# VectorE's order around the low half of h: ahead of the routing table, and ahead of the scaling of the tile before

## The chip, the core and the metric

The kernel runs on one core of a Trainium2 chip. The time is the device time of one execution in microseconds (us). Five engines work side by side, each through its own list of instructions in order: TensorE (PE in the profile; its weight loads are PEld), VectorE (DVE), ScalarE (ACT), GpSimd (POOL) and SyncE (SP). They wait for each other on semaphores only. A queue named with a q (SPq, DVEq, POOLq) is the part of an engine that handles registers, branches, waits and the start of transfers.

## What is computed

A retention layer, a gated feed-forward layer, and a mixture of experts with one expert per token. What matters here is the third:

```
logits = x @ w_gate;  e_idx = argmax(logits)
gate_w = softmax(logits)[e_idx];  eom = sigmoid(x @ w_output_gate)
for each expert e:
    h  = relu(x[rows of e] @ w1[e])
    ye = h @ w2[e]
    out[rows of e] = gate_w * eom[:, e] * ye
```

There are 3072 tokens of width 512, 8 experts and 1024 hidden columns in an expert. All matrices are float32. Each float32 product is made of three products in a shorter format: a factor is split into a high part (a cast) and a low part (the value less its high part), and high by high, high by low and low by high are added up.

## The kernel before

The tokens are sorted by expert into tiles of 128 rows. Tile 0 and tile 1 run with expert 0 while the sorting goes on; from tile 2 on, the order comes from a table (`tile_tab`) that VectorE writes in `dve_route`. Which expert a tile uses, and whether the next one changes it, is read from that table into registers. In this data 27 tiles run, 0 to 26, and the expert changes 7 times.

One tile i goes like this, with the names of the code:

- GpSimd gathers its 128 rows into `xg` by an indirect DMA (`gather`, L1367), from indices in `idx_gather`.
- PE transposes them (`x_T`, L663) into bank 4. VectorE splits the result into high and low (`split_xe`, L675 and L677) and copies the rows' scale (`keep_scale`, L667, semaphore `scale_kept`).
- PE multiplies by w1 (`up`, L1427, 24 matmuls) into banks 0 and 1; ScalarE applies the relu (L1293).
- PE transposes h (`h_T`, L1435) into banks 2 and 3, in two halves. ScalarE casts each half to `hT_hi` (L1298, semaphore `hT_hi_done`). VectorE computes `hT_lo`, in two halves too (`hT_rest`, L1162, semaphore `hT_lo_done`).
- PE multiplies by w2 (`down`, L1451, 24 matmuls in 8 groups of three) into bank 5 or 6 by turns. It may start when half 0 of `hT_lo` is there, needs half 1 in the middle, and needs that bank free (`ye_read` of the tile two before).
- VectorE scales the rows into `ye` (`scale_y`, L1332), and GpSimd scatters them to the output (`scatter`, L1372). `scale_y` waits for the end of the `down` of its tile (`ye_done`) and for a free half of `ye` (`ye_free`).

PE's order is skewed: h_T(i), up(i+1), x_T(i+2), down(i), h_T(i+1), and so on. So the low part of tile i is wanted only after an `up`, save at two places where there is no `up` between them:

- Tile 1, during the routing. PE's order is down(0), the first half of the sort (`pe_sort`, L1153), the rest of down(0), h_T(1), the second half of the sort (semaphore `slots_done`), down(1). The `x_T` of tile 2 stands inside down(1), ahead of its last group of three.
- The last tile, 26. PE's order is down(25), with h_T(26) inside, then at once down(26). The low and high parts of this tile have buffers of their own (`hT_last`).

VectorE's loop over the tiles is in pairs. In `in_pairs` pairs 1 to 11 run in a loop, and the rest (pairs 12 to 15) in a second loop, where each pair stands under a test (`pairs > m`). With 13 pairs in this data the last three are skipped, and VectorE's queue goes through the loop's registers and branches for them (L1252, L1253).

When a tile changes the expert, ScalarE and VectorE also split the new weights (`split_w1` and `split_w2`, L700 and L703). SyncE loads them (L721): it may start when the table is written (`route_done`) and when GpSimd has asked for the gathers of tiles 2, 3 and 4 (`rows_asked`). The gather of tile 4 waits for `scale_kept` of tile 2, since it writes to the same buffer.

Of the kernel before, what the change touches and what calls it, by code (L numbers as in the profile page):

```python
# [88 lines left out]
def build(nc, steps_in, weights_in, gates_in, w1_in, w2_in, const_in, xT_dram, x_dram, out):  # L89
# [12 lines left out]
    def place(name, shape, dt=F32, where=None):  # L102

        offset = at[0] if where is None else where
        t = nc.alloc_sbuf_tensor_at(name, list(shape), dt, offset=offset)
        after = (offset + int(np.prod(shape[1:])) * 4 + 31) // 32 * 32
        assert after <= nc.sbuf_usable_end, (name, after)
        if where is None:
            at[0] = after
        return t.ap()  # L110
# [114 lines left out]
    hT_hi = place("hT_hi", (P, KE, P), F32R)  # L225
# [5 lines left out]
    hT_lo = place("hT_lo", (P, KE, P), F32R)  # L231
# [422 lines left out]
    ye_done, ye_read, ye_free, last_ye = sem("ye_done"), sem("ye_read"), sem("ye_free"), sem("last_ye")  # L654
# [14 lines left out]
    def split_xe(dve, i, s):  # L669
        dve.wait_ge(xe_T_done, i + 1)  # L670
        if isinstance(i, int) and i < FIRST:
            keep_scale(i, xg_first[s])
        at_bank = {0: 3, 1: 2}.get(i, 4) if isinstance(i, int) else 4
        psum = bank[at_bank].rearrange("p (k t) -> p k t", k=KD)
        nc.vector.tensor_copy(xe_hi[:, s], psum).then_inc(xe_done, 1)  # L675
        dve.wait_ge(xe_done, 2 * i + 1)
        nc.vector.tensor_tensor(xe_lo[:, s], psum, xe_hi[:, s].bitcast(F32), ALU.subtract).then_inc(xe_done, 1)  # L677
        if not (isinstance(i, int) and i < FIRST):
            keep_scale(i, xg[s])
# [28 lines left out]
    def split_w2(eng, hi, run, parts=range(PARTS)):  # L708
        split_weight(eng, hi, run, raw2, raw2_in, w2_hi, w2_lo, W2_SPAN, w2_hi_done, w2_lo_done, parts)
# [112 lines left out]
    def on_pe(g):  # L822
        return g - (GROUPS - 2)
# [33 lines left out]
    def dve_partial(dve, g, part=part_sb):  # L857
        dve.wait_ge(part_done, on_pe(g) + 1)
        nc.vector.tensor_copy(part, apart(g)).then_inc(part_read, 1)
# [20 lines left out]
    def linker(dve, base, link_done=link_done):  # L880

        count = [0]

        def link(ins):
            count[0] += 1
            ins.then_inc(link_done, 1)
            dve.wait_ge(link_done, base + count[0])

        return link, count
# [265 lines left out]
        if half == 1:  # L1155
            ins.then_inc(slots_done, 1)

    def hT_rest(dve, i, hT=(hT_hi, hT_lo)):
        high, low = hT
        for o in range(2):  # L1160
            dve.wait_ge(hT_hi_done, 2 * i + o + 1)
            nc.vector.tensor_tensor(low[:, 4 * o:4 * o + 4].rearrange("p k t -> p (k t)"), bank[2 + o],  # L1162
                                    high[:, 4 * o:4 * o + 4].rearrange("p k t -> p (k t)").bitcast(F32),
                                    ALU.subtract).then_inc(hT_lo_done, 1)

    def dve_route(dve):
        v = nc.vector
        known = LAST * TG
        link, count = linker(dve, LINKED)
        split_w2(dve, False, 0, (0, 1))  # L1170
        split_xe(dve, 1, 1)
        for t in range(TG):
            dve.wait_ge(yT_done, TG * on_pe(LAST) + t + 1)
            v.tensor_copy(yT_last[:, :, t * P:(t + 1) * P], bank[4 + t].rearrange("p (k t) -> p k t", k=KD)).then_inc(yT_read, 1)
        split_w2(dve, False, 0, (2,))
        dve_partial(dve, LAST, part_last)
        split_w2(dve, False, 0, (3,))
        dve_logits(dve, LAST)
        dve_choose(dve, LAST, link)
        dve_gate(dve, LAST, link)  # L1180
        dve_scale(dve, LAST, link)
        hT_rest(dve, 0)

        dve.wait_ge(rank_done, GROUPS)
        link(v.tensor_scalar(e_cnti, bank[7][:, COUNT:COUNT + NE], float(P - 1), None, ALU.add))
        link(v.tensor_scalar(e_tli, e_cnti, 7, None, ALU.logical_shift_right))
        link(v.tensor_copy(e_tiles, e_tli))
        src = e_tiles
        for dst, shift in ((e_s1, 1), (e_s2, 2), (e_end, 4)):
            v.tensor_copy(dst[:, 0:shift], src[:, 0:shift])  # L1190
            link(v.tensor_tensor(dst[:, shift:], src[:, shift:], src[:, 0:NE - shift], ALU.add))
            src = dst
        link(v.tensor_tensor(e_base, e_end, e_tiles, ALU.subtract))
        dve_rank(dve, LAST, link)

        dve_off_hot(dve, known, TILES)
        link(v.tensor_tensor(base8, onehot, under(e_base, TILES), ALU.mult))
        link(v.tensor_reduce(t_base, base8, AX.X, ALU.add))
        link(v.tensor_tensor(t_base, t_base, t_tle, ALU.add))

        link(v.tensor_tensor(tile_eq, under(iota[:, 0:COLS], TILES), over(t_base, COLS), ALU.is_equal))
        v.tensor_tensor(tile_hot, tile_eq, over(id1, COLS), ALU.mult).then_inc(hot_done, 1)

        v.tensor_scalar(e_used, e_tiles, 0.0, None, ALU.is_gt)
        link(v.tensor_scalar(e_s1[:, 0:1], e_end[:, NE - 1:NE], -1.0, None, ALU.add))
        link(v.tensor_scalar(tl_i, iota[:, 0:COLS + 1], e_s1[:, 0:1], None, ALU.min))
        link(v.tensor_tensor(tl_cmp, under(e_end, COLS + 1), over(tl_i, NE), ALU.is_le))
        link(v.tensor_tensor(tl_cmp2, tl_cmp, under(e_used, COLS + 1), ALU.mult))

        dve.wait_ge(slots_done, 1)  # L1210
        v.tensor_scalar(idx_gather[:, FIRST:], bank[7][:, FIRST:COLS], -1.0, 0.0, ALU.add, ALU.max).then_inc(gather_ready, 1)
        v.tensor_copy(inv, bank[7][:, 0:COLS])

        v.tensor_reduce(tl_e, tl_cmp, AX.X, ALU.add)
        link(v.tensor_reduce(tl_run, tl_cmp2, AX.X, ALU.add))
        link(v.tensor_tensor(tl_new, tl_run[:, 1:COLS + 1], tl_run[:, 0:COLS], ALU.subtract))

        dve.wait_ge(x_out, 16 * GROUPS)
        link(v.tensor_copy(pair_i, e_end[:, NE - 1:NE]))
        v.tensor_scalar(n_pairs, pair_i, 1, None, ALU.logical_shift_right)  # L1220
        v.tensor_copy(tile_tab[:, :, 0], tl_e[:, 0:COLS])
        v.tensor_copy(tile_tab[:, :, 1], tl_run[:, 0:COLS])
        v.memset(tile_tab[:, 0:1, 2], 1)
        v.tensor_copy(tile_tab[:, 1:COLS, 2], tl_new[:, 0:COLS - 1])
        v.tensor_copy(tile_tab[:, :, 3], tl_new).then_inc(route_done, 1)

        hT_rest(dve, 1)
        v.tensor_scalar(inv_e, inv, 0.0, float(2 * NT), ALU.is_equal, ALU.mult)
        link(v.tensor_scalar(inv_s, inv, -1.0, None, ALU.add))
        link(v.tensor_tensor(inv_s, inv_s, inv_e, ALU.add))  # L1230
        link(v.tensor_copy(idx_scatter, inv_s))
        last = dve.value_load(n_pairs[0:1, 0:1], min_val=PAIRS_MIN, max_val=PAIRS_MAX)
        v.tensor_scalar(n_before, n_pairs, -1, None, ALU.add)
        v.tensor_copy(idx_last, idx_scatter[:, bass.ds(last * 2, 1)]).then_inc(scatter_ready, 1)
# [93 lines left out]
    def dve_experts(dve):  # L1328
        def scale_y(i, s):
            dve.wait_ge(ye_done, i + 1)  # L1330
            dve.wait_ge(ye_free, i - 1 + 2)
            return nc.vector.tensor_scalar(ye[:, s], bank[5 + s], slot_scale[:, bass.ds(i, 1)], None, ALU.mult)  # L1332

        def tile(i, s):
            with dve.If(entry(dve, i, NEW_NEXT) == 1):
                split_w1(dve, False, entry(dve, i, RUN) + 1)
            if not isinstance(i, int):
                split_xe(dve, i + 1, 1 - s)
            with dve.If(entry(dve, i, NEW_HERE) == 1):
                split_w2(dve, False, entry(dve, i, RUN))  # L1340
            scale_y(i - 1, 1 - s).then_inc(ye_read, 1)

        def pair(m):
            hT_rest(dve, 2 * m)
            tile(2 * m + 1, 1)
            hT_rest(dve, 2 * m + 1)
            tile(2 * m + 2, 0)

        split_xe_early(dve, 2, 0)
        split_xe(dve, 3, 1)  # L1350
        with dve.If(entry(dve, 1, NEW_NEXT) == 1):
            split_w1(dve, False, 1)
        scale_y(0, 0).then_inc(ye_read, 1)
        tile(2, 0)
        pairs = dve.value_load(n_pairs[0:1, 0:1], min_val=PAIRS_MIN, max_val=PAIRS_MAX)
        in_pairs(dve, pairs, pair)
        hT_rest(dve, pairs * 2, hT_last)
        scale_y(pairs * 2, 0).then_inc(last_ye, 1)


# [216 lines left out]
```

## Time and profile before

| | us |
|---|---|
| median of 3 runs | 1047.63 (1045.71 to 1048.64) |
| the profiled execution | 1046.8, its span 1045.0 |
| PE busy | 1017.6 (97% of the span) |
| VectorE busy | 554.5 (53%) |
| ScalarE busy | 283.6 (27%) |
| GpSimd busy | 112.4 (11%) |
| share of PE in the chain that ended last | 96% |

The span is the time from the first to the last instruction of the profiled execution; 1.8 us of its time lie around the span. The granted clock is the share of TensorE's full clock that it was given: 1.00 stands for 2.4 GHz and 0.50 for 1.2 GHz.

### The profile page before, as it was taken

How to read it: one execution, taken by the hardware profiler on the slowest of the kernel's cores; microseconds unless marked ns; L12 is line 12 of the kernel's file. 1: busy time of each engine (PE TensorE's matmuls, PEld its weight loads, DVE VectorE, ACT ScalarE, POOL GpSimd, SP SyncE). 2: the span in 40 equal slices, each digit the busy share in tenths (PEclk: the TensorE clock that was granted, in tenths of full speed). 3: DMA queues.
4: the chain of work that ended last, by engine and by line, in shares of the span. 5: the costliest groups of instructions: out<-in, count | busy, mean ns of one | idle time of the engine just before them, and what ended most of it. 6: DMA issues, size and time to landing. Idle time of an engine off the chain costs nothing.

```text
span 1045.0 us, 17350 instructions
## 1 busy us (share of the span) xinstructions
PE 1017.6 (97%) x5761; PEld 844.9 (81%) x5762; DVE 554.5 (53%) x1211; ACT 283.6 (27%) x490; POOL 112.4 (11%) x108
## 2 busy tenths in 40 slices
PE   6989999999999999999999999998999999999996
PEld 5878888888888888888888878887888888888885
DVE  3444333487557747773877223474554545445541
ACT  2534332221112122112211212130534433334330
POOL 4780000000000000000000000001121111111111
PEclk9999999999999999999999999999999999999999
DMA  9998800511051114104210212011753435253311
GB/s 364 368 295 249 223 1 1 139 53 48 4 151 51 41 34 129 53 28 99 73 51 21 81 41 81 11 51 42 281 193 133 144 105 167 74 192 120 118 36 36
DMA packets 53874, 114.50 MB, mean 110 GB/s; under 512 B 8750, under 2 KB 23406, under 8 KB 53297
## 3 DMA queue, kind: packets, MB, share of 16 engines
q1 hardware_dynamic: 48752, 98.95, 30.1%
q0 software_dynamic: 4480, 13.91, 4.0%
q8 instruction: 38, 0.62, 0.2%
q10 hardware_dynamic: 576, 0.79, 0.2%
q14 instruction: 28, 0.22, 0.1%
HBM read 96.81 MB, written 17.61 MB: 109 GB/s over the span
## 4 chain that ended last, share of the span: by engine, by line
PE 96%; DMA 2%; issue 1%; DVE 1%; ACT 0%; POOL 0%; ACTq 0%; DVEq 0%; POOLq 0%
PE bank L1077 38%; PE bank L1097 19%; PE bank L1427 15%; PE bank L1451 14%; PE bank L1435 2%; PE bank L604 2%; PE bank L555 2%; PE bank L663 1%; PE bank L569 1%; PE bank L590 1%; DMA rows<-in_steps 1%; DMA qdec_t<-in_consts 1%; PE bank L1153 0%; PE bank L977 0%; PE bank L844 0%
## 5 line engine op out<-in xcount | busy, mean ns | idle before, releaser
L1077 PE MATMUL bank<-x_hi,wab_hi 128*128 128x512 f32 x576 | 224.4, 390 | 0.0
L1077 PE MATMUL bank<-x_hi,wab_lo 128*128 128x512 f32 x576 | 224.1, 389 | 0.0
L1077 PE MATMUL bank<-x_lo,wab_hi 128*128 128x512 f32 x576 | 224.1, 389 | 0.0
L999 DVE SCALAR_TENSOR_TENSOR products<-y_sb,gate_row 128x512 f32<-128x512 f32 x256 | 176.8, 691 | 22.7 <-DMA gate_row<-xT_dram 15.3
L1427 PE MATMUL bank<-w,xe 128*128 (+1 forms) x648 | 158.9, 399 | 0.5 <-DVE xe L687 0.5
L1011 DVE TENSOR_TENSOR g_sb<-bank,b_sb 128x512 f32<-128x512 f32 x72 | 49.7, 690 | 175.3 <-PE bank L1077 175.3
L1427 PEld LDWEIGHTS bank<-w,xe 128*128 128x128 f32 x648 | 119.3, 188 | 28.2 <-issue 1.8
L1077 PEld LDWEIGHTS bank<-x_hi,wab_hi 128*128 128x128 f32 x576 | 108.1, 188 | 22.7 <-issue 0.2
L1077 PEld LDWEIGHTS bank<-x_hi,wab_lo 128*128 128x128 f32 x576 | 108.1, 188 | 22.4
L1077 PEld LDWEIGHTS bank<-x_lo,wab_hi 128*128 128x128 f32 x576 | 108.2, 188 | 22.3
L1097 PE MATMUL bank<-wo_hi,g_hi 128*128 128x512 f32 x288 | 113.4, 394 | 0.0
L1097 PE MATMUL bank<-wo_hi,g_lo 128*128 128x512 f32 x288 | 112.2, 390 | 0.0
L1097 PE MATMUL bank<-wo_lo,g_hi 128*128 128x512 f32 x288 | 112.1, 389 | 0.0
L789 ACT CAST g_hi<-g_sb 128x512 fp32r<-128x512 f32 x72 | 44.7, 621 | 231.0 <-DVE g_sb L1011 231.0
L787 ACT COPY b_sb<-bank 128x512 f32<-128x512 f32 x72 | 42.3, 587 | 214.1 <-PE bank L1077 214.1
L1367 POOL DMA_INDIRECT xg<-x_rows,idx_gather x28 | 29.2, 1043 | 649.8 <-DVE idx_gather L969 597.7
L1451 PE MATMUL bank<-w_hi,hT_hi 128*128 (+1 forms) x208 | 84.3, 405 | 2.8 <-DVE hT_lo L1162 2.8
L1451 PE MATMUL bank<-w_hi,hT_lo 128*128 (+1 forms) x208 | 82.0, 394 | 0.0
L1451 PE MATMUL bank<-w_lo,hT_hi 128*128 (+1 forms) x208 | 81.6, 393 | 0.0
L1013 DVE TENSOR_TENSOR g_lo<-g_sb,g_hi 128x512 fp32r<-128x512 f32 x72 | 49.8, 692 | 49.5 <-ACT g_hi L789 49.5
L1097 PEld LDWEIGHTS bank<-wo_hi,g_hi 128*128 128x128 f32 x288 | 54.1, 188 | 11.7 <-issue 0.8
L1097 PEld LDWEIGHTS bank<-wo_hi,g_lo 128*128 128x128 f32 x288 | 54.1, 188 | 11.5
(172 smaller groups left out, 1052.7 us busy)
## 6 DMA issues: line engine op xcount, KB each, us to landing
raw<-in_w SPq DMA_DIRECT2D x64, 512.0 KB, 7.9
gate_row<-xT_dram SPq DMA_DIRECT2D x64, 256.0 KB, 3.2
rows<-in_steps SPq DMA_DIRECT2D x20, 768.0 KB, 8.3
rows<-in_steps SPq DMA_DIRECT2D x24, 256.0 KB, 7.6
wab_raw<-in_weights SPq DMA_DIRECT2D x24, 256.0 KB, 9.0
x_rows<-y_sb SPq DMA_DIRECT2D x6, 1024.0 KB, 8.6
xT_dram<-x_all SPq DMA_DIRECT2D x4, 1024.0 KB, 11.5
x_raw<-xT_dram SPq DMA_DIRECT2D x16, 256.0 KB, 8.0
```

Source lines behind the costliest of these rows:

```text
L555: ins = nc.tensor.matmul(bank[2 * i + o][:, cols], kT[half_p, cols], qT[half_p, cols], start=True, stop=True)
L604: ins = nc.tensor.matmul(out_at(i, p, o), rows[:, c, 3, h * D:(h + 1) * D], probs[j][:, i, h, :], start=False, stop=(i == ROUND - 1 and p ...
L787: nc.scalar.copy(b_sb[:, f % 2], b_bank(f)).then_inc(b_read, 1)
L789: nc.scalar.copy(g_hi[:, f % 2], g_sb[:, f % 2]).then_inc(g_hi_done, 1)
L999: nc.vector.scalar_tensor_tensor(products, y_sb[:, t], 1.0, gate_row[e % GATE_SLOTS], ALU.mult, ALU.mult, accum_out=L3[:, t, e:e + 1]).the ...
L1011: nc.vector.tensor_tensor(g_sb[:, f % 2], a_bank(f), b_sb[:, f % 2], ALU.mult).then_inc(g_done, 1)
L1013: nc.vector.tensor_tensor(g_lo[:, f % 2], g_sb[:, f % 2], g_hi[:, f % 2].bitcast(F32), ALU.subtract).then_inc(g_lo_done, 1)
L1077: ins = nc.tensor.matmul(to, wab(w, f, j), x[s][:, k, :], start=(k == 0 and m == 0), stop=(k == KD - 1 and m == 2))
L1097: ins = nc.tensor.matmul(bank[4 + t], gp[:, f % 2, toks], wo(w, f), start=(f == 0 and m == 0), stop=(f == KF - 1 and m == 2))
L1367: nc.gpsimd.indirect_dma_start(out=xg_first[s] if i < FIRST else xg[s], out_offset=None, in_=x_rows[0:rows_there], in_offset=bass.Indirect ...
L1427: ins = nc.tensor.matmul(bank[o], x[:, s, k, :], w[:, bass.ds(half + (k * FE + o * 512), 512)], start=(k == 0 and m == 0), stop=(k == KD - ...
L1451: ins = nc.tensor.matmul(bank[5 + s], h[:, k, :], w[:, bass.ds(half + k * DM, DM)], start=(k == 0 and m == 0), stop=(k == KE - 1 and m == 2))
```

## The change

Nothing is added and nothing taken out: two kinds of instruction take another place in VectorE's list. In the routing, the two halves of `hT_rest` of tile 1 stood behind the last write of the table. Half 0 now stands ahead of the wait for the sort (`slots_done`), and half 1 right behind the instruction that writes `idx_gather`. In the expert loop `scale_y(i - 1)` was the last step of `tile(i)`, so it stood ahead of `hT_rest` of tile i. Now it stands behind it, and ahead of the splits of the tile after. The last two scalings follow the last `hT_rest`.

```diff
-    def hT_rest(dve, i, hT=(hT_hi, hT_lo)):
+    def hT_rest(dve, i, hT=(hT_hi, hT_lo), halves=range(2)):
         high, low = hT
-        for o in range(2):
+        for o in halves:
...
+        hT_rest(dve, 1, halves=(0,))
         dve.wait_ge(slots_done, 1)
         v.tensor_scalar(idx_gather[:, FIRST:], bank[7][:, FIRST:COLS], -1.0, 0.0, ALU.add, ALU.max).then_inc(gather_ready, 1)
+        hT_rest(dve, 1, halves=(1,))
         v.tensor_copy(inv, bank[7][:, 0:COLS])
...
         v.tensor_copy(tile_tab[:, :, 3], tl_new).then_inc(route_done, 1)
 
-        hT_rest(dve, 1)
         v.tensor_scalar(inv_e, inv, 0.0, float(2 * NT), ALU.is_equal, ALU.mult)
...
             with dve.If(entry(dve, i, NEW_HERE) == 1):
                 split_w2(dve, False, entry(dve, i, RUN))
-            scale_y(i - 1, 1 - s).then_inc(ye_read, 1)
 
         def pair(m):
             hT_rest(dve, 2 * m)
+            scale_y(2 * m - 1, 1).then_inc(ye_read, 1)
             tile(2 * m + 1, 1)
             hT_rest(dve, 2 * m + 1)
+            scale_y(2 * m, 0).then_inc(ye_read, 1)
             tile(2 * m + 2, 0)
...
         in_pairs(dve, pairs, pair)
         hT_rest(dve, pairs * 2, hT_last)
+        scale_y(pairs * 2 - 1, 1).then_inc(ye_read, 1)
         scale_y(pairs * 2, 0).then_inc(last_ye, 1)
```

VectorE's list around the sort, before the change. L1208 is the last step that needs nothing from the sort, L1211 writes the gather's indices, L1225 is the last write of the table, L1228 begins the scatter's indices:

```order
L1208 TENSOR_TENSOR tl8_1_158<-tl8_0_157,e_5_80 128x280 [waits link_done]
L1211 TENSOR_SCALAR idx_gather_52<-bank7 128x32 [waits slots_done,link_done]
L1212 COPY inv_0_150<-bank7 128x34
...
L1225 CAST tile_tab_136<-inv_3_153 128x34
L1162 TENSOR_TENSOR hT_lo_133<-bank2,hT_hi_131 128x512 [waits hT_hi_done]
L1162 TENSOR_TENSOR hT_lo_133<-bank3,hT_hi_131 128x512 [waits hT_hi_done]
L1228 TENSOR_SCALAR inv_1_151<-inv_0_150 128x34
```

The same place after the change (L1212 now writes the gather's indices, L1227 is the last write of the table):

```order
L1208 TENSOR_TENSOR tl8_1_158<-tl8_0_157,e_5_80 128x280 [waits link_done]
L1162 TENSOR_TENSOR hT_lo_133<-bank2,hT_hi_131 128x512 [waits hT_hi_done,link_done]
L1212 TENSOR_SCALAR idx_gather_52<-bank7 128x32 [waits slots_done]
L1162 TENSOR_TENSOR hT_lo_133<-bank3,hT_hi_131 128x512 [waits hT_hi_done]
L1214 COPY inv_0_150<-bank7 128x34
...
L1227 CAST tile_tab_136<-inv_3_153 128x34
L1229 TENSOR_SCALAR inv_1_151<-inv_0_150 128x34
```

One half passes the whole table and the wait for the sort; the other stays behind the index write and passes the rest of the table.

The end of VectorE's list before the change. Bank 6 holds the result of tile 25 and bank 5 that of tile 26; L1253 and L1252 are the loop over pairs:

```order
L1332 REGISTER_ALU [waits ye_free,ye_done]
L1332 TENSOR_SCALAR ye_134<-bank6,slot_scale_54 128x512
L1253 UNCONDITIONAL_BRANCH
L1252 REGISTER_ALU
L1252 COMPARE_AND_BRANCH
L1161 ISA
L1162 TENSOR_TENSOR hT_last_lo_145<-bank2,hT_last_hi_144 128x512 [waits hT_hi_done]
L1161 REGISTER_ALU
L1162 TENSOR_TENSOR hT_last_lo_145<-bank3,hT_last_hi_144 128x512 [waits hT_hi_done]
```

And after it:

```order
L1253 REGISTER_ALU
L1253 COMPARE_AND_BRANCH
L1161 ISA
L1162 TENSOR_TENSOR hT_last_lo_145<-bank2,hT_last_hi_144 128x512 [waits hT_hi_done]
L1161 REGISTER_ALU
L1162 TENSOR_TENSOR hT_last_lo_145<-bank3,hT_last_hi_144 128x512 [waits hT_hi_done]
L1333 ISA [waits ye_free,ye_done]
L1333 TENSOR_SCALAR ye_134<-bank6,slot_scale_54 128x512
```

The loop's branches and the low part of the last tile no longer stand behind the wait for the end of down(25).

## Rows read from the trace of the kernel before

**Rows 1.** Waits of PE from 600 us on: us in total, times, longest.

```profile
PE bank L1451 <- DVE hT_last_lo L1162: 3.5, 1, 3.5
PE bank L1451 <- DVE hT_lo L1162: 2.8, 1, 2.8
```

**Rows 2.** Timeline around down(1): start us, duration us, instruction, [idle before, releaser].

```profile
711.26 1.07 ACT L1298 CAST hT_hi<-bank 128x512 fp32r<-128x512 f32 x2 [6.67 <-PE bank L1435]
...
713.02 0.19 DVE L1211 TENSOR_SCALAR idx_gather<-bank 128x32 int32<-128x32 f32 x1 [3.46 <-PE bank L1153]
...
714.05 0.99 POOL L1367 DMA_INDIRECT xg<-x_rows,idx_gather  x1 [35.55 <-DVE idx_gather L1211]
...
714.92 0.68 DVE L1162 TENSOR_TENSOR hT_lo<-bank,hT_hi 128x512 fp32r<-128x512 f32 x1
...
715.35 1.00 POOL L1367 DMA_INDIRECT xg<-x_rows,idx_gather  x1 [0.31 <-issue]
...
715.66 0.50 PE L1451 MATMUL bank<-w_hi,hT_hi 128*128 128x512 f32 x1 [2.75 <-DVE hT_lo L1162]
...
722.14 0.60 PE L663 MATMUL bank<-ident,xg 128*128 128x128 f32 x4
...
723.97 2.37 PE L1427 MATMUL bank<-w,xe 128*128 x9 [0.53 <-DVE xe L687]
```

**Rows 3.** Timeline of one tile of the loop whose successor changes the expert.

```profile
805.20 0.75 DVE L1332 TENSOR_SCALAR ye<-bank,slot_scale 128x512 f32<-128x512 f32 x1 [4.11 <-PE bank L1451]
805.54 1.07 ACT L1298 CAST hT_hi<-bank 128x512 fp32r<-128x512 f32 x2 [5.77 <-PE bank L1435]
...
806.16 1.29 DVE L1162 TENSOR_TENSOR hT_lo<-bank,hT_hi 128x512 fp32r<-128x512 f32 x2 [0.21 <-ACT hT_hi L1298]
...
808.96 4.63 DVE L703 TENSOR_TENSOR w<-raw,w 128x1024 f32 x4 [1.51 <-ACT w L700]
...
811.73 0.48 PE L1451 MATMUL bank<-w_hi,hT_hi 128*128 x1
...
814.23 0.69 DVE L677 TENSOR_TENSOR xe<-bank,xe 128x512 fp32r<-128x512 f32 x1
...
817.29 1.04 PE L1435 MATMUL bank<-ident,h_sb 128*128 128x128 f32 x8
```

**Rows 4.** Busy time, clock and DMA by stretch: PE, PEld, DVE, ACT, POOL, PEclk, DMA share, GB/s.

```profile
717.00:719.00 2.00, 2.00 (x6) 1.52 (x6) 0.29 (x2) 0.00 (x0) 0.00 (x0) 0.50 0.48 129
```

**Rows 5.** The gather of tile 2, from its issue at 714.05: median us to landing.

```profile
xg<-x_rows,idx_gather POOLq DMA_INDIRECT x1, 3.4
```

**Rows 6.** Timeline of the gather of tile 4, the first weight loads, and up(4).

```profile
725.30 1.00 POOL L1367 DMA_INDIRECT xg<-x_rows,idx_gather  x1 [8.95 <-DVE slot_scale L667]
...
729.30 4.76 SPq L721 DMA_DIRECT2D raw<-in_w  x8
...
741.66 0.69 DVE L677 TENSOR_TENSOR xe<-bank,xe 128x512 fp32r<-128x512 f32 x1
...
743.77 5.85 PE L1427 MATMUL bank<-w,xe 128*128 x24
```

**Rows 7.** Timeline of the end, from the last h_T on.

```profile
1026.74 1.07 ACT L1298 CAST hT_last_hi<-bank 128x512 fp32r<-128x512 f32 x2 [4.00 <-PE bank L1435]
...
1028.82 0.40 PE L1451 MATMUL bank<-w_hi,hT_lo 128*128 x1
...
1029.35 0.75 DVE L1332 TENSOR_SCALAR ye<-bank,slot_scale 128x512 f32<-128x512 f32 x1 [5.30 <-PE bank L1451]
...
1031.70 1.29 DVE L1162 TENSOR_TENSOR hT_last_lo<-bank,hT_last_hi 128x512 fp32r<-128x512 f32 x2 [1.60 <-issue]
...
1032.77 0.49 PE L1451 MATMUL bank<-w_hi,hT_last_hi 128*128 x1 [3.55 <-DVE hT_last_lo L1162]
...
1039.72 0.39 PE L1451 MATMUL bank<-w_hi,hT_last_lo 128*128 x1
```

**Rows 8.** Busy time, clock and DMA of one stretch of down(26).

```profile
1034.00:1037.00 3.00, 3.00 (x9) 2.32 (x8) 0.00 (x0) 0.00 (x0) 0.00 (x0) 0.50 0.00 0
```

## The prediction

> **What bounds the kernel now.** I read the chain that ended last first: 96% of it is PE, so only what lets PE start earlier, or run faster, is worth time. Then the waits of PE in the expert part: two of them are on the low part of h, 3.5 us at the last tile and 2.8 us at tile 1 [rows 1]. Then the timelines around these two, to see what VectorE did meanwhile, and the granted clock behind each. The reader is to see that in both places VectorE has the low part standing behind something that it doesn't need: behind the routing table at tile 1 [rows 2], behind the end of down(25) and the loop's branches at tile 26 [rows 7]. In the loop proper PE waits for nothing.
>
> **Place 1, tile 1.** Before, the sort ends at 712.91 (715.66 less the idle 2.75), and PE waits for half 0 of the low part, which runs from 714.92 to 715.60 [rows 2].
> After, half 0 needs only ScalarE's first cast. In the loop the low part starts 0.62 after the pair of casts (805.54 to 806.16) [rows 3]; the pair begins here at 711.26 [rows 2], so half 0 runs from 711.88 to 712.56. VectorE is idle then (3.46 us up to 713.02), so the index write stays at 713.02 and the gather at 714.05. Half 1 follows at about 713.13 and is there at 713.8, while PE wants it 12 matmuls in, near 715.5. Half 0 is there some 0.3 us before the sort ends; down(1) follows the sort, and the stall of 2.75 goes.
> A second term is the clock. In down(1) it stands at 0.50 (1.2 GHz) in the stretch read [rows 4], behind a stall of 2.75. Its 21 matmuls up to x_T(2) take 722.14 - 715.66 = 6.48 us. At full clock 24 take 817.29 - 811.73 = 5.56 [rows 3], 0.23 each, so 21 take 4.87. That is 1.61 saved if PE, now not idle, keeps 2.4 GHz.
> What is late next: x_T(2) would stand at 712.91 + 4.87 = 717.78, by the ends, or some 0.2 earlier, since matmuls overlap. The gather of tile 2 lands 3.4 us behind 714.05, at 717.45 [rows 2, 5]. That is just in time; between nothing and 0.3 us are lost there, and I take 0.1. Place 1 gives 2.75 + 0.2 (overlap) + 1.61 - 0.1 = 4.5 us.
> What follows has to come forward too. The table is written 0.6 us later than before, by one low half (half 1) ahead of it (713.13 to 713.8), but PE, SyncE and ScalarE want it only behind x_T(2). The scatter's indices come 0.6 us earlier, as half 0 now lies in the idle time. The weight loads begin at 729.30, behind the gather of tile 4 at 725.30, which itself waited 8.95 us for the scale of tile 2 [rows 6]. That chain starts from x_T(2), so it shifts with PE. With it goes the tightest margin I found, up(4): its x is split until 741.66 + 0.69 = 742.35, and PE starts at 743.77, 1.4 us later [rows 6]. The margin stays 1.4 if both move.
>
> **Place 2, the last tile.** Before, VectorE waits for the end of down(25), scales at 1029.35, goes through the branches of three skipped pairs, and starts the low part at 1031.70; PE starts down(26) at 1032.77 [rows 7]. After, VectorE's last step ends at 1024.05 (1029.35 less its idle 5.30). The branches take at most 1031.70 - 1029.35 = 2.35 us, and the table load ahead of them at most 0.75 (the idle 1.51 ahead of a split of w1 holds two of them [rows 3]), so its queue is through by 1027.15. ScalarE's casts begin at 1026.74, so half 0 may start at 1027.36 and ends at 1028.04. Down(25)'s last matmul starts at 1028.82, so down(26) can start one step (0.23) later, at 1029.05: 1032.77 - 1029.05 = 3.72 us.
> The clock again: 0.50 in the middle of down(26) [rows 8]. First to last matmul takes 1039.72 - 1032.77 = 6.95; at full clock 23 steps of 5.56/24 are 5.33. That saves 1.62. The scaling of tile 25 still starts at 1029.35, when down(25) ends, with nothing ahead of it; its scatter is out long before the last one. Place 2 gives 3.72 + 1.62 = 5.3 us, and all of it reaches the end, since behind down(26) stand only one scaling and one scatter.
>
> **The loop.** In the loop's tiles `scale_y` goes behind the low part. VectorE waited there for the end of down, and then for ScalarE's cast by another 0.21 [rows 3], so the low part does not come earlier, and the scaling comes some 2.2 us later (807.4 for 805.2). Behind it stands the split of w1, ahead of which VectorE is idle for 1.51, part of that with register work of its own [rows 3]: I put its delay at 0.2, and at 0.75 (the whole scaling) at most. The x split behind it ends at 814.92 and the next up starts behind the transposes of 817.29, 2.4 us later or more: covered. The scatter goes 2.2 us later, and behind it a gather that PE wants more than a tile later; a tile is 12.1 us (805.20 to 817.29): covered. Bank 5 or 6 is wanted again two tiles on. I put the loop at 0, between 0.2 gained and 1 lost.
>
> **The sum.** 4.5 + 5.3 = 9.8 us. The profiled execution took 1046.8, so it would be 1037.0. The median of the runs is 0.8 above that execution: 1037.8.
>
> **Bounds.** Place 1: at least 2.75 - 0.5, if the clock falls anyway and x_T(2) waits half a microsecond; at most 4.7. Place 2: at least 3.55 (no gain of clock), at most 5.4. Sum between 5.8 and 10.1, plus or minus 1 for the median of three runs, which lay 2.9 apart.
>
> **A rule against it.** Gather 3 was issued at 715.35 and took GpSimd 1.00, while the low part ran on VectorE (714.92 to 716.2); gather 2 took 0.99 with only small steps beside it, and gather 4 at 725.30 took 1.00 [rows 2, 6]. So in this trace GpSimd does not wait for the low part. The Trainium skill ("SBUF — State Buffer", section "SBUF: two separate sides") says that VectorE and GpSimd share one pair of ports as an exclusive lock, and that a DMA issued by GpSimd can starve for descriptors while VectorE runs an operation that holds both. By that rule half 1, now at 713.1 to 713.8, could hold back gather 2; the trace does not agree, since the same operation beside gather 3 cost it 0.00 to 0.01.
>
> **Rivals.**
> *A. x_T(2) becomes the wait.* The gather's landing (717.45) and x_T(2) (717.6 to 717.8) are all but equal, and the index write or GpSimd's start may slip by up to one low half (0.68). PE then stands for up to 0.7, and with the wait of 0.53 before up(2) [rows 2] close behind, the clock may fall as it did before: 1.6 lost. Gain 9.8 - 0.7 - 1.6 = 7.5: 1040.1. For it: no margin. Against: nothing of before is ahead of the index write that is not idle time now.
> *B. The loads do not come forward.* If the first expert's weights hang on something else than tile 2's scale, PE comes 4.5 us early to up(4) with 1.4 of margin, waits 3.1, and loses 1.6 of clock: place 1 gives nothing, the sum is 5.3 to 5.1: 1042.4. Against: the 8.95 us wait of gather 4 on that scale [rows 6].
> *C. Slower.* The place is VectorE ahead of the w1 split in the 7 tiles that bring a new expert. If the scaling there had to wait for `ye_free` (its scatter two tiles before not landed), the split and the x split behind it would be late. From the point where this exceeds 2.4 us, up waits, say 0.5, each time with 1.6 of clock: 7 x (0.5 + 1.6) = 14.7, so 1037.8 + 14.7 = 1052.5. Against: the scalings shown waited for PE, 4.11 and 5.30 us, and not for a scatter [rows 3, 7]; the scatter now has 2.2 us less out of two tiles, 24.
> *D. Only one place works*, for instance the last low part is still late because VectorE's queue is: 9.8 less about 5 gives 1042.8.
>
> **How the numbers follow.** The forecast, both places whole: 0.72, 1037.8, by itself 1036.3 to 1039.3. A: 0.14. B: 0.05. C: 0.02. D: 0.05. Nothing changed at all: 0.02. A measurement of this kernel can tell about 0.3%, 3.1 us, from no change: faster means under 1044.5. The forecast, A, B and D lie below that, less a little for a mis-sized B or D: 0.95 faster, 0.035 same, 0.015 slower. The range reaches over A: 1035.8 to 1041.0.
>
> **What would show it.** Right: no wait of PE on a low part of h from 600 us on; granted clock 1.00 through down(1) and down(26); x_T(2) near 717.6 and the index write still near 713.0; weight loads starting near 724.8; down(26) starting one step behind down(25); the span 9.8 shorter, about 4.5 of it by 740 us. Wrong: a wait of PE at x_T(2) on the gather, or at up(4) on the weights; clock of 0.50 in either place; up waiting in the loop.

## The result and the profile after

The changed kernel takes 1037.36 us (median of 5 runs, 1037.05 to 1041.24), against 1047.63 of the kernel before (5 runs, 1045.71 to 1048.64). The ratio is 0.9914, with a 95% interval of 0.9893 to 0.9936: faster by 9.0 us, between 6.7 and 11.2. The ratio goes by all runs and not by the medians, which lie 10.3 apart. The profiled execution took 1037.36, its span is 1035.5. The forecast was 1037.8.

Waits of PE from 600 us on, kernel after:

```profile
PE bank L1430 <- DVE xe L687: 0.5, 1, 0.5
PE bank L1438 <- ACT h_sb L1294: 0.3, 1, 0.3
PE bank L1454 <- issue: 0.2, 1, 0.2
```

Both waits on a low part [rows 1] are gone. What is left is small: 0.5 at up(2), 0.3 at one h_T, and 0.2 on "issue", which is new.

Timeline of the kernel after around down(1) (start, duration, instruction, [idle before, releaser]):

```profile
711.60 1.07 ACT L1299 CAST hT_hi<-bank 128x512 fp32r<-128x512 f32 x2 [6.67 <-PE bank L1438]
711.76 1.49 PE L1153 MATMUL bank<-tile_hot,off_hot 128*128 128x34 f32 x12
712.29 0.69 DVE L1162 TENSOR_TENSOR hT_lo<-bank,hT_hi 128x512 fp32r<-128x512 f32 x1 [2.38 <-ACT hT_hi L1299]
713.10 0.48 PE L1454 MATMUL bank<-w_hi,hT_hi 128*128 128x512 f32 x1
713.29 0.19 DVE L1212 TENSOR_SCALAR idx_gather<-bank 128x32 int32<-128x32 f32 x1 [0.30 <-PE bank L1153]
713.40 0.68 DVE L1162 TENSOR_TENSOR hT_lo<-bank,hT_hi 128x512 fp32r<-128x512 f32 x1
...
714.33 0.99 POOL L1370 DMA_INDIRECT xg<-x_rows,idx_gather  x1 [35.45 <-DVE idx_gather L1212]
...
718.00 0.60 PE L663 MATMUL bank<-ident,xg 128*128 128x128 f32 x4
...
719.83 2.37 PE L1430 MATMUL bank<-w,xe 128*128 x9 [0.53 <-DVE xe L687]
...
721.16 1.00 POOL L1370 DMA_INDIRECT xg<-x_rows,idx_gather  x1 [4.53 <-DVE slot_scale L667]
...
725.15 4.67 SPq L721 DMA_DIRECT2D raw<-in_w  x8
```

Half 0 runs in what was idle time, down(1) follows the sort with no gap, and half 1 lies behind the index write, beside matmuls. The 21 matmuls up to x_T(2) take 718.00 - 713.10 = 4.90 us, for 6.48 before [rows 2]. The gather of tile 4 waits 4.53 for the scale of tile 2 instead of 8.95, and the weight loads begin at 725.15 for 729.30 [rows 6].

The end of the kernel after:

```profile
1022.75 1.08 ACT L1299 CAST hT_last_hi<-bank 128x512 fp32r<-128x512 f32 x2 [4.16 <-PE bank L1438]
...
1023.37 1.29 DVE L1162 TENSOR_TENSOR hT_last_lo<-bank,hT_last_hi 128x512 fp32r<-128x512 f32 x2 [3.46 <-ACT hT_last_hi L1299]
...
1024.84 0.40 PE L1454 MATMUL bank<-w_hi,hT_lo 128*128 x1
1025.07 0.39 PE L1454 MATMUL bank<-w_hi,hT_last_hi 128*128 x1
...
1025.38 0.75 DVE L1333 TENSOR_SCALAR ye<-bank,slot_scale 128x512 f32<-128x512 f32 x1 [0.72 <-PE bank L1454]
...
1030.29 0.39 PE L1454 MATMUL bank<-w_hi,hT_last_lo 128*128 x1
```

The low part starts 0.62 behind ScalarE's casts, as in the loop; down(26) starts 0.23 behind the last matmul of down(25) instead of 3.95 (1028.82 to 1032.77 [rows 7]). The clock in both places (columns as in rows 4):

```profile
713.00:718.00 5.00, 5.00 (x25) 4.08 (x25) 3.44 (x19) 0.00 (x0) 2.00 (x2) 1.00 0.30 74
1025.00:1030.00 5.00, 5.00 (x23) 4.13 (x23) 0.75 (x1) 0.00 (x0) 1.00 (x1) 1.00 0.14 52
```

It is 1.00 (2.4 GHz), where rows 4 and 8 had 0.50 (1.2 GHz).

**A ruler that leaves out the start.** Up to the second half of the sort all kernels of this study have the same instructions in the same order, and yet it starts anywhere from 709.77 to 712.77 in their traces. So I compare from its start (the L1153 row) to the end of the span: 1045.0 - 711.42 = 333.58 before, 1035.5 - 711.76 = 323.74 after. That is 9.84 us less, good to about 0.1, since the span is given to a tenth. It is made up of these pieces: from the sort to up(2) 12.55 before (711.42 to 723.97) and 8.07 after, 4.48 less; from the last matmul of down(25) to the last of down(26) 10.90 before and 5.45 after, 5.45 less; and about 0.1 is lost again between and behind them.

### The profile page after: what moved, and what is told of

It is laid out like the page before. It is cut to its first block, busy times and chain, and to the rows that moved or that the text cites. A ratio compares the mean times of both kernels' runs of the same rounds, so it can differ in the third digit from the quotient of the medians.

```text
span 1035.5 us, 17351 instructions
## 1 busy us (share of the span) xinstructions
PE 1014.7 (98%) x5761; PEld 843.4 (81%) x5762; DVE 553.4 (53%) x1211; ACT 283.6 (27%) x490; POOL 118.3 (11%) x108
## 4 chain that ended last, share of the span: by engine, by line
PE 96%; DMA 3%; issue 0%; POOL 0%; ACT 0%; DVE 0%; ACTq 0%; POOLq 0%; DVEq 0%
PE bank L1077 38%; PE bank L1097 19%; PE bank L1430 15%; PE bank L1454 14%; PE bank L1438 2%; DMA rows<-in_steps 2%; PE bank L604 2%; PE bank L555 2%; PE bank L663 1%; PE bank L569 1%; PE bank L590 1%; DMA qdec_t<-in_consts 1%; PE bank L1153 0%; PE bank L977 0%; PE bank L844 0%
## 5 line engine op out<-in xcount | busy, mean ns | idle before, releaser
L1370 POOL DMA_INDIRECT xg<-x_rows,idx_gather x28 | 35.1, 1252 | 646.2 <-DVE idx_gather L969 598.6
L1162 DVE TENSOR_TENSOR hT_lo<-bank,hT_hi 128x512 fp32r<-128x512 f32 x52 | 33.5, 685 | 73.7 <-ACT hT_hi L1299 73.7
```

The lines of the kernel that those rows point to most:

```text
L1370: nc.gpsimd.indirect_dma_start(out=xg_first[s] if i < FIRST else xg[s], out_offset=None, in_=x_rows[0:rows_there], in_offset=bass.Indirect ...
```

## The experiments

Four kernels split the change. A second set puts it under strain, and a third looks at what was left.

| kernel | median us | ratio to before (95%) | sort to end |
|---|---|---|---|
| before | 1047.63 | | 333.58 |
| after | 1037.36 | 0.9914 (0.9893 to 0.9936) | 323.74 |
| route_only | 1041.98 | 0.9952 (0.9939 to 0.9965) | 330.23 |
| loop_and_end | 1042.96 | 0.9958 (0.9942 to 0.9974) | 329.16 |
| end_only | 1041.44 | 0.9940 (0.9927 to 0.9953) | 328.99 |
| loop_only | 1043.48 | 0.9965 (0.9954 to 0.9977) | 330.47 |
| after_again | 1038.71 | 0.9917 (0.9899 to 0.9936) | 323.90 |
| route_and_end | 1036.62 | 0.9897 (0.9880 to 0.9914) | 323.54 |
| late_index | 1039.16 | 0.9913 (0.9893 to 0.9934) | 326.90 |
| loads_late | 1045.38 | 0.9976 (0.9959 to 0.9993) | 330.53 |
| load_early | 1036.31 | 0.9904 (0.9887 to 0.9922) | 323.32 |
| best | 1036.38 | 0.9903 (0.9888 to 0.9919) | 323.38 |
| both_ahead | 1037.31 | 0.9918 (0.9898 to 0.9938) | 323.81 |
| before_again | 1046.04 (one run) | | 333.08 |

The kernels route_only to loop_only ran on one chip, after_again to loads_late on a second, load_early to before_again on a third; each ratio is to the kernel before on the same chip. "Sort to end" is that of the one profiled execution of each.

### The change taken apart

**route_only**: the moves in `dve_route` alone.

```diff
+        hT_rest(dve, 1, halves=(0,))
         dve.wait_ge(slots_done, 1)
         v.tensor_scalar(idx_gather[:, FIRST:], ...)
+        hT_rest(dve, 1, halves=(1,))
...
-        hT_rest(dve, 1)
```

> Only the low part of tile 1 is moved (half 0 ahead of the wait for the sort, half 1 behind the index write); loop and end as before. Theory (the two places are separate, each gives its stall plus the loss of clock behind it): 4.1 to 4.5 us less than before, about 1043.2; no wait of PE at down(1), granted clock 1.00 there; the wait of 3.5 us at down(26) and the clock of 0.50 behind it as before. Rival (the places are not separate, or the end gives all of it): 0 to 2 us less.

Measured: 0.9952, 5.0 us less. From sort to up(2) 8.07 us (709.77 to 717.84), as in the kernel after. But sort to end is only 3.35 less than before, since the untouched end cost more this time: the same stall, and a longer slow stretch behind it. The end of route_only:

```profile
1022.65 0.40 PE L1452 MATMUL bank<-w_hi,hT_lo 128*128 x1
1026.60 0.79 PE L1452 MATMUL bank<-w_hi,hT_last_hi 128*128 x1 [3.55 <-DVE hT_last_lo L1162]
...
1034.75 0.39 PE L1452 MATMUL bank<-w_hi,hT_last_lo 128*128 x1
```

8.15 us from first to last matmul, for 6.95 before and 5.22 after. Place 1 is worth its 4.5 by itself.

**loop_and_end**: the moves in `dve_experts` alone; `hT_rest(dve, 1)` stands where it stood.

> The routing is as before; only the scaling is moved behind the low part, in the loop and at the end. Theory: 5.3 us less than before, about 1042.3; wait of 2.75 us at down(1) and clock 0.50 behind it as before; none at down(26). Rival (the gain at the end is only the stall, the clock falls all the same): 3.7 us less.

Measured: 0.9958, 4.4 us less. At the end 5.45 us, as in the kernel after (1030.52 to 1035.97). At down(1) the stall is 2.75 again, and its 21 matmuls take 7.33 us (716.28 to 723.61), for 6.48 before.

**end_only**: the loop keeps its old order; the new one only at the last pair of neighbours.

```diff
         def pair(m):
+            scale_y(2 * m - 1, 1).then_inc(ye_read, 1)
             hT_rest(dve, 2 * m)
             tile(2 * m + 1, 1)
+            scale_y(2 * m, 0).then_inc(ye_read, 1)
             hT_rest(dve, 2 * m + 1)
...
-            scale_y(i - 1, 1 - s).then_inc(ye_read, 1)
...
         hT_rest(dve, pairs * 2, hT_last)
+        scale_y(pairs * 2 - 1, 1).then_inc(ye_read, 1)
```

> The routing as before, the order in the loop as before (scaling of tile i-1 ahead of the low part of tile i), but the scaling of tile 25 behind the low part of tile 26: only the last pair of neighbours changes places. Theory (the loop's new order is worth nothing, the end is worth all): the same as loop_and_end within 0.3 us, 5.3 us less than before. Rival (the loop's order gives or costs something, by the split of w1 0.2 to 0.75 us later in 7 tiles, say): differs from loop_and_end by 1 us or more.

Measured: 0.9940, 6.3 us less; 5.45 at the end again (1029.35 to 1034.80). By the traces the loop's new order is worth nothing: sort to end is 0.17 less than in loop_and_end. The medians differ by 1.5, as the rival had it, but the two intervals overlap, and of the 1.17 between the two profiled executions (1041.88 and 1043.05) 1.03 lie ahead of the change, where the second half of the sort starts at 711.01 here and at 712.04 there.

**loop_only**: loop_and_end with the last two steps in the old order, so that only the branches of the skipped pairs come ahead.

```diff
-        hT_rest(dve, pairs * 2, hT_last)
         scale_y(pairs * 2 - 1, 1).then_inc(ye_read, 1)
+        hT_rest(dve, pairs * 2, hT_last)
         scale_y(pairs * 2, 0).then_inc(last_ye, 1)
```

> The routing as before; in the loop the scaling is behind the low part, but at the end the scaling of tile 25 stands ahead of the low part of tile 26, behind the loop's branches. Theory: the branches (2.35 us at most) are now done while PE works; the low part waits for the end of down(25), the scaling and ScalarE's cast that is long done, so PE's stall falls from 3.5 to about 1.5 us (scaling from 1029.35, low part 0.65 behind it, 0.7 long, 0.37 to PE). If the clock falls behind a stall of this length as it did behind 2.75 and 3.55, the gain is 2 us; if it does not, 2 + 1.6 = 3.6 us. Rival (the branches don't move, the whole gain came from the place of the scaling): no gain.

Measured: 0.9965, 3.7 us less. The end of loop_only, and the clock of two stretches behind the stall:

```profile
1028.86 0.75 DVE L1332 TENSOR_SCALAR ye<-bank,slot_scale 128x512 f32<-128x512 f32 x1 [5.54 <-PE bank L1453]
1029.53 1.28 DVE L1162 TENSOR_TENSOR hT_last_lo<-bank,hT_last_hi 128x512 fp32r<-128x512 f32 x2
...
1030.59 0.49 PE L1453 MATMUL bank<-w_hi,hT_last_hi 128*128 x1 [1.88 <-DVE hT_last_lo L1162]
...
1035.92 0.39 PE L1453 MATMUL bank<-w_hi,hT_last_lo 128*128 x1
```

```profile
1030.60:1033.00 2.40, 2.40 (x11) 1.99 (x12) 0.20 (x1) 0.00 (x0) 0.81 (x1) 1.00 0.29 109
1033.00:1036.00 3.00, 3.00 (x15) 2.42 (x13) 0.00 (x0) 0.00 (x0) 0.00 (x0) 1.00 0.00 0
```

The stall is 1.88, for about 1.5 expected, and the clock stays at 1.00: down(26) takes 5.33. So the 5.45 us of the end are, by these rows: 1.67 the branches (3.55 less 1.88), 2.05 the wait for the scaling and what it leads to (the rest of the 3.72), and 1.7 the clock (6.95 less 5.22).

### The change under strain

**after_again**: the kernel after, once more.

> The kernel after the change once more, beside the three below on one chip. About 1037.4; from the start of the second half of the sort (L1153) to the end of the span 323.7 us as in its first trace (before: 333.6).

Measured: 0.9917; sort to end 323.90, 0.16 from the first trace.

**late_index**: the index write later.

```diff
-        v.tensor_scalar(idx_gather[:, FIRST:], ...).then_inc(gather_ready, 1)
         hT_rest(dve, 1, halves=(1,))
         v.tensor_copy(inv, bank[7][:, 0:COLS])
         v.tensor_reduce(tl_e, tl_cmp, AX.X, ALU.add)
         link(v.tensor_reduce(tl_run, tl_cmp2, AX.X, ALU.add))
+        v.tensor_scalar(idx_gather[:, FIRST:], ...).then_inc(gather_ready, 1)
```

> The kernel after, with the write of idx_gather moved behind both low halves, the copy of inv and the two reductions, so 1.5 us later (714.8 for 713.3). Theory (x_T(2) in down(1) has a margin of 0.3 us on the gather of tile 2, which lands 3.3 us behind its issue): PE waits 1.1 to 1.3 us at x_T(2), and everything behind shifts by that; if the clock falls behind it, 1.6 to 2.8 us more, so 1038.6 or 1040.2 to 1041.4. Rival (the real margin is larger, the landing is earlier than the profile has it): under 0.5 us.

Measured: by its median no different from after_again, by the trace 3.0 us longer from sort to end (326.90 for 323.90). Timeline and clock of late_index:

```profile
710.80 1.49 PE L1153 MATMUL bank<-tile_hot,off_hot 128*128 128x34 f32 x12
...
713.86 0.19 DVE L1217 TENSOR_SCALAR idx_gather<-bank 128x32 int32<-128x32 f32 x1
714.90 1.00 POOL L1370 DMA_INDIRECT xg<-x_rows,idx_gather  x1 [37.00 <-DVE idx_gather L1217]
...
718.38 0.66 PE L663 MATMUL bank<-ident,xg 128*128 128x128 f32 x4 [1.18 <-DMA xg<-x_rows,idx_gather]
720.36 3.91 PE L1430 MATMUL bank<-w,xe 128*128 x9 [0.64 <-DVE xe L687]
```

```profile
718.40:720.30 1.90, 1.32 (x7) 0.85 (x7) 1.18 (x3) 0.00 (x0) 0.00 (x0) 1.00 0.29 112
720.40:724.00 3.60, 3.60 (x9) 2.89 (x10) 0.40 (x2) 0.00 (x0) 1.00 (x1) 0.53 0.17 34
```

The index write comes 3.06 behind the start of the sort's second half for 1.53 in the kernel after, 1.53 late; PE stands for 1.18 at x_T(2), so 0.35 of the delay does not show as idle time there. That is not free time, though: up(2) starts 9.56 behind the sort (720.36 less 710.80) for 8.07, 1.49 later, so it had a margin of 0.04 only. Behind the second wait, at up(2), the clock falls, and its first nine matmuls take 3.91 for 2.37. This is rival A as a kernel, with more than twice the 0.68 us of delay that A allows for: 1.49 + 1.54 = 3.0, all of it. The trace is of the slowest of its four executions (1039.54). Its granted clock was 0.998 over the whole span and 0.999 to 1.000 in the other three, so whether the clock fell behind up(2) in those too is open.

**both_ahead**: both low halves ahead of the wait for the sort (`hT_rest(dve, 1)` there, and nothing behind the index write).

> The kernel after, with both low halves of tile 1 ahead of the wait for the sort. Half 1 then runs from about 0.6 us behind half 0, and ends about 0.3 us behind the sort; the index write and the gather are 0.2 to 0.3 us later. Theory (margin at x_T(2) 0.3 us): PE waits 0 to 0.2 us there, the table is written 0.5 us earlier, which nothing needs; no difference from after. Rival (any delay of the index write reaches PE in full and pulls the clock down): 1.6 us or more slower.

Measured: 0.9918, sort to end 323.81. PE in both_ahead:

```profile
711.69 1.49 PE L1153 MATMUL bank<-tile_hot,off_hot 128*128 128x34 f32 x12
...
717.85 0.43 PEld L663 LDWEIGHTS bank<-ident,xg 128*128 128x128 f32 x4 [0.20 <-DMA xg<-x_rows,idx_gather]
...
719.93 2.35 PE L1429 MATMUL bank<-w,xe 128*128 x9 [0.72 <-DVE xe L687]
```

The index write is 0.21 later (1.74 behind the sort's start for 1.53), PE's weight load at x_T(2) waits 0.20 on the gather, and up(2) starts 8.24 behind the sort for 8.07, 0.17 later: again a margin of 0.04. By the end of the span this can't be told from the kernel after (323.74 and 323.90), so the place of half 1 is worth 0.2 us at most.

**loads_late**: SyncE is let loose behind the first scatter.

```diff
         gather(4)
-        pool.sem_inc(rows_asked, 1)
...
             scatter(1 - i % 2, idx_scatter[:, i - 1:i])
+            if i == 1:
+                pool.sem_inc(rows_asked, 1)
```

> The kernel after, but SyncE is let loose (rows_asked) only behind the scatter of tile 0, 4.8 us later (about 727.0 for 722.2). Nothing else moves. Theory (the first expert's weights have 1.4 us of margin at up(4), where x of tile 4 is split 738.2 and up(4) starts at 739.6, since both start from x_T(2)): up(4) is late by about 3.4 us, plus 1.6 to 2.8 if the clock falls; 1040.8 to 1043.6. Rival (the margin is much wider, the loads don't bound that split): no change.

Measured: 0.9976, only 2.5 us below the kernel before; sort to end 330.53, 6.8 more than after. PE in loads_late, and the x split of tile 4 on VectorE:

```profile
719.01 0.60 PE L663 MATMUL bank<-ident,xg 128*128 128x128 f32 x4
...
742.51 1.15 PE L1439 MATMUL bank<-ident,h_sb 128*128 128x128 f32 x8 [2.53 <-ACT h_sb L1294]
...
745.18 8.24 PE L1431 MATMUL bank<-w,xe 128*128 x24 [1.52 <-DVE xe L677]
```

```profile
744.04 0.69 DVE L677 TENSOR_TENSOR xe<-bank,xe 128x512 fp32r<-128x512 f32 x1
```

The first weight loads in loads_late, then up(4) in the kernel after (the view ends ahead of its last matmul):

```profile
731.25 14.40 SPq L721 DMA_DIRECT2D raw<-in_w  x12
```

```profile
739.62 5.61 PE L1430 MATMUL bank<-w,xe 128*128 x23
```

The x split of tile 4 ends 25.72 behind x_T(2) here (744.73 less 719.01) and 20.24 in the kernel after (738.24 less 718.00), 5.48 later; PE stands for 2.53 + 1.52 = 4.05, and up(4) starts 26.17 behind x_T(2) for 21.62, 4.55 later. So 0.93 us of the delay was free. The margin of 1.4 that the prediction and I read, from the end of the split to the start of up(4), is there (738.24 to 739.62), but 0.45 of it is what up(4) took to start behind the split even when it waited for it (744.73 to 745.18). The loads start 5.1 later, counted from x_T(2) (12.24 behind it for 7.15), near the 4.8 I had put down. The wait shows at two places, since ScalarE's relu of tile 3 is queued behind its weight casts, and h_T(3) waits for the relu. Up(4) then takes 8.24 for 5.85 [rows 6]. The median, 1045.38, lies above the 1040.8 to 1043.6 that I expected: the split was 0.7 later, and the margin 0.45 less, than I had reckoned with. This is rival B as a kernel, its loads 5.1 late where B has them 4.5 late: it took all of place 1 and more.

### What was left

**route_and_end**: route_only and end_only together.

> Both places of the change, but the loop keeps its old order (scaling of tile i-1, then the low part of tile i); only the scaling of tile 25 is behind the low part of tile 26. Theory (the loop's new order makes nothing faster; it moves GpSimd's gather 3 us later, onto PE's register load of n_before ahead of down(25), which then took 0.53 for 0.32 us and let PE stand 0.25): 0.1 to 0.3 us less than after_again from sort to end, 323.5; the load takes 0.32 again, its medians the same within noise. Rival (the 0.25 is chance): no difference, and the load is slow here too.

Measured: 0.9897; sort to end 323.54. The register load of PE (columns: count, min/median/max ns, start), first in route_and_end, then in the kernel after:

```profile
L1505 PEldq TENSOR_LOAD <-n_before x1: 322/322/322, 1015.3 to 1015.3; - x1
```

```profile
L1505 PEldq TENSOR_LOAD <-n_before x1: 537/537/537, 1017.1 to 1017.1; - x1
```

What lies around it in the kernel after:

```profile
1016.64 1.04 POOL L1370 DMA_INDIRECT xg<-x_rows,idx_gather  x1 [0.30 <-issue]
...
1018.59 0.49 PE L1454 MATMUL bank<-w_hi,hT_hi 128*128 x1 [0.20 <-issue]
```

In the five traces with the old loop order and the load at this place it takes 318 to 322 ns, in the seven with the new order 521 to 547. In the new order the scaling is later, with it GpSimd's scatter, and with that the gather behind it, which then lies on PE's load.

**load_early**: the kernel after with that load far ahead.

```diff
+        pe.wait_ge(scatter_ready, 1)
+        n_last = pe.value_load(n_before[0:1, 0:1], ...)
         to_next_pair(0, even, odd)
...
-        pe.wait_ge(scatter_ready, 1)
-        n = pe.value_load(n_before[0:1, 0:1], ...)
```

> The kernel after, with PE's register load of n_before (and its wait for scatter_ready) moved from ahead of down(25) to ahead of the first tiles of the loop, 300 us earlier, where PE's list is full. Theory (PE stood 0.20 to 0.26 us ahead of down(25) because this load took 0.53 us there beside GpSimd's gather): no wait ahead of down(25), from x_T(27) to down(25) 0.36 us as in the other tiles (0.80 in the kernel after, 0.64 before), sort to end 0.4 us less than after (323.4). Rival (the wait there is the loop's exit, not the load): 0.6 to 0.8 us stay.

Measured: 0.9904; sort to end 323.32, 0.42 less than after. PE ahead of down(25) in load_early:

```profile
1017.25 0.60 PE L663 MATMUL bank<-ident,xg 128*128 128x128 f32 x4
1017.60 0.49 PE L1454 MATMUL bank<-w_hi,hT_hi 128*128 x1
```

0.35 from x_T(27) to down(25), for 0.80 in the kernel after and 0.64 before. So the load did hold PE up there. That the gather beside it makes it slow is borne out by twelve traces, but not by a kernel in which the gather alone was moved.

**best**: route_and_end with the early load.

> route_and_end with the same early load: both places of the change, the loop's old order, the load out of the way. Theory: sort to end 323.3, the least of all; its median about 0.3 us below route_and_end, which is below what runs can tell, so 1036.5 to 1037.5. Rival (the load costs as much at its new place): as route_and_end.

Measured: 0.9903 (0.9888 to 0.9919), the same as load_early and route_and_end within their intervals; 323.38. The three can't be told apart, and none is shown to beat the kernel after.

**before_again**: a second trace of the kernel before.

> The kernel before once more, for a second trace of its two stalls. Theory (the stalls are fixed by the order, 2.75 and 3.55 us, but how long the clock stays at 0.50 behind each is not): stalls within 0.1 us of the first trace; the 21 matmuls of down(1) up to x_T(2) take 6.5 to 7.5 us (6.48 in the first trace), down(26) from its first to its last matmul 6.9 to 8.2 (6.95). Rival (the clock's loss is fixed by the stall): 6.48 and 6.95 again.

Measured: the stalls are 2.75 and 3.55 again, to the hundredth. Behind them the 21 matmuls take 6.25 (715.36 to 721.61) and down(26) 6.93: the first below the range I gave.

## Why the prediction was right, point by point

**What bounds.** Right: PE's two waits on the low part were all that the change could reach, and both went.

**Place 1.** Right in each term. Half 0 was forecast 0.62 behind the casts and came 0.69 behind (711.60 to 712.29); the index write kept its place (1.53 behind the start of the sort's second half, for 1.60 before); the gather's landing and x_T(2) were forecast within 0.3 of each other, and the margin at up(2) is 0.04, so it was nearly missed. The 0.1 us that I charged there was not paid. The table, forecast 0.6 later, came 0.5 later (its last write starts 3.91 behind the sort for 3.42), and nothing waited for it. Forecast 4.5, measured 4.48.

**Place 2.** Right: 5.3 forecast, 5.45 measured, just past the 5.4 that it gave as the most. I had the start of down(26) one step behind down(25) and VectorE's queue through in time; both hold.

**The clock.** The terms, 1.61 and 1.62, are right for the execution that they were read from. As a property of the change they are too narrow: behind the same stall of 2.75 the 21 matmuls took 6.25, 6.48, 6.52, 7.33 and 7.43 us in five traces, for 4.90 without it, so the clock costs 1.35 to 2.53; behind 3.55 down(26) took 6.93, 6.95 and 8.15 for 5.22, 1.71 to 2.93. What I took for a constant is a draw, and the two draws of the profiled execution were low ones. That the sum came out within 0.1 is in part luck: the five traces with the stall at place 1 average 6.80 there and the three at place 2 7.34, and from such draws the same change would have given 10.5. The Trainium skill ("TensorE: Matmul & The Clock Gate", section "What's actually happening") says of the start of a kernel that the number of matmuls which one and the same kernel runs at the lower clock differs from run to run, and gives 6, 11 and 14. The traces show the same in kind behind a stall in the middle, with a spread of 1.2 us at both places.

**What has to come forward.** Right: the weight loads went from 729.30 to 725.15 and from the end of the x split to up(4) it is still 1.4 (738.24 to 739.62). Of this 0.93 was free time, by loads_late. That kernel also shows that place 1 would have been lost had the loads not come forward.

**The loop.** Nearly right: 0 forecast. The delay of the w1 split, put at 0.2, did not come: the split starts 4.05 behind h_T in both kernels (804.91 to 808.96 and 800.77 to 804.82). What I had not seen is 0.16 us more at PE's load of n_before: I followed the later scatter to the gather and to the tile that needs it, and not to what else runs beside that gather.

**The rule of the port.** Gather 2, with half 1 ending 0.25 ahead of it (714.08), took GpSimd 0.99 and landed 3.3 us behind its issue, for 0.99 and 3.4 before. Nothing was held back, but the two did not run side by side either, so this does not test the rule. The rows with a low half beside a gather's issue are those of gather 3 before the change [rows 2], which took 1.00.

**The rivals.** A was near: up(2) had a margin of 0.04, and late_index, with 1.53 us of delay, cost 3.0 in its trace, where A had 2.3 for 0.7. loads_late, with loads 5.1 late, cost 6.8, where B had 4.7 for 4.5. C and D did not show: no `up` waited in the loop.

## What to carry to other kernels

A stall on the bounding engine costs its length, and here from nothing (behind 1.88 us) up to 2.9 us more for the clock behind it, so look at the pitch of the matmuls that follow a wait, and not at the wait alone. In the list of an in-order engine, look for a step that is wanted soon and stands behind one that waits for something else: the end of another tile, a table, or merely the branches of a loop's skipped rounds. Ask of each gain whether the transfers behind it start from the same event; here they did, and a kernel in which they did not lost 6.8 us. To learn how much of a margin is free, delay the step on purpose and compare the starts of what follows: idle time alone gave 0.35 where 0.04 was free, and the gap in the timeline 1.4 where 0.93 was. And when small changes are compared, read the traces from a common point behind the part that varies, and remember that each is one execution: the trace of late_index is 3 us longer than that of after_again, while the medians of the two differ by 0.45.

## What the runs showed of the hardware

- The clock fell behind stalls of 2.75 us (five traces) and 3.55 us (three), and not behind one of 1.88. But it did fall behind two short ones, 1.18 and 0.64, with four transposes and three matmuls between them (late_index), and not behind the single one of 0.72 in both_ahead. In loads_late it fell during the eight transposes behind a stall of 2.53 (1.00 from 742.50 to 743.20, 0.50 from 743.70 on).
- How long it stays at 0.50 behind one and the same stall varies: 1.35 to 2.53 us lost behind 2.75, and 1.71 to 2.93 behind 3.55.
- A register load on PE took 0.32 us alone and 0.52 to 0.55 with GpSimd issuing an indirect DMA at the same time (five traces against seven; that the one causes the other was not tested by itself).
- Fourteen traces of kernels with the same instructions up to the sort reach its second half over a range of 3.0 us.
